# Moving the products of gates ("merges") of a gated linear attention from GpSimd to VectorE

## The reference

```python
# q, k, v, f_logit: (4 batches, 8 heads, 768 tokens, 48)
f = 1.0 / (1.0 + np.exp(-f_logit))
for t in range(S):
    state = f[:, :, t, :, None] * state + einsum('bhd,bhe->bhde', k[:, :, t], v[:, :, t])
    y[:, :, t] = einsum('bhd,bhde->bhe', q[:, :, t], state)
x = y as (3072 tokens, 384)
# first layer, w_in 384 x 2048, w_out 2048 x 384
h = x @ w_in
g = where(h >= 1, h, where(h <= -1, 0, (h + 1)**2 / 4))
x = g @ w_out
# second layer, w_gate and w_val 384 x 1536, w_out 1536 x 384
out = (silu(x @ w_gate) * (x @ w_val)) @ w_out
```

## Time and profile before

| | before |
|---|---|
| median of 3 runs | 1084.7 us (1084.14 to 1085.7) |
| profiled execution: its time | 1084.7 us |
| its span in the trace | 1082.9 us |
| PE busy | 1013.7 us, 94% |
| DVE busy | 539.7 us, 50% |
| ACT busy | 454.3 us, 42% |
| POOL busy | 449.7 us, 42% |
| POOL merges (L890) | 80 instructions, 44.1 us |

### The profile page before, as it was taken

How to read it: one execution, slowest core, us unless ns; L and a number is a source line. 1 busy time by engine, 2 the same in 40 slices (tenths; PEclk the granted TensorE clock), 3 DMA queues, 4 the chain that set the end, 5 groups by cost and what they waited for, 6 DMA issues and landing times.

```text
span 1082.9 us, 19234 instructions
## 1 busy us (share of the span) xinstructions
PE 1013.7 (94%) x7816; PEld 828.0 (76%) x7816; DVE 539.7 (50%) x743; ACT 454.3 (42%) x840; POOL 449.7 (42%) x368
## 2 busy tenths in 40 slices
PE   1484999999999999999999999999999999999997
PEld 1473778778777877877788888888888888888886
DVE  3965894885688388659736532222223222232221
ACT  6456647544753665375336532222122221222221
POOL 1856982764475366537526522212121221212121
PEclk9666999999999999999999999999999999999999
DMA  9323005202400600130043100010010010000000
GB/s 358 153 86 130 1 2 166 79 2 75 159 13 2 215 31 1 44 115 30 2 176 131 45 30 30 1 59 1 1 59 1 1 59 1 30 1 1 30 1 29
DMA packets 17367, 63.52 MB, mean 59 GB/s; under 512 B 1920, under 2 KB 2176, under 8 KB 16512
## 3 DMA queue, kind: packets, MB, share of 16 engines
q1 hardware_dynamic: 17280, 62.30, 15.9%
HBM read 52.85 MB, written 9.44 MB: 58 GB/s over the span
## 4 chain that ended last, share of the span: by engine, by line
PE 85%; issue 5%; ACT 4%; DVE 3%; POOL 2%; DMA 0%; POOLq 0%; ACTq 0%; SPq 0%; DVEq 0%
PE acc L447 11%; PE acc L448 10%; PE acc L449 10%; PE bank L474 7%; PE bank L473 7%; PE bank L475 7%; PE bank L346 6%; PE hid L433 6%; PE hid L434 5%; PE hid L435 5%; ACT scores L527 2%; PE hid L474 2%; PE hid L475 2%; PE hid L473 2%; PE bank L378 2%
## 5 line engine op out<-in xcount | busy, mean ns | idle before, releaser
L929 POOL TENSOR_TENSOR g_lo<-prod,g_hi 128x512 fp32r<-128x512 f32 x72 | 93.1, 1293 | 347.4 <-ACT g_hi L652 347.4
L922 POOL TENSOR_TENSOR g_lo<-act_tmp,g_hi 128x512 fp32r<-128x512 f32 x96 | 140.0, 1459 | 182.0 <-ACT g_hi L613 182.0
L827 DVE TENSOR_TENSOR sig<-sig,bank 128x512 f32<-128x512 f32 x72 | 49.5, 688 | 275.4 <-ACT sig L646 275.4
L740 DVE COPY_PREDICATED scores<-mask,bank 64x512 f32<-64x512 int32 x144 | 134.5, 934 | 32.7 <-PE bank L346 31.0
L652 ACT CAST g_hi<-prod 128x512 fp32r<-128x512 f32 x72 | 44.7, 621 | 247.8 <-PE acc L449 247.8
L433 PE MATMUL hid<-x_hi,win_hi 128*128 128x512 f32 x288 | 119.1, 414 | 16.1 <-DVE act_tmp L815 16.1
L882 POOL TENSOR_TENSOR keys<-keys,gates 128x512 f32<-128x512 f32 x82 | 108.0, 1317 | 57.5 <-PE bank L346 46.1
L613 ACT CAST g_hi<-act_tmp 128x512 fp32r<-128x512 f32 x96 | 59.5, 620 | 166.0 <-DVE act_tmp L815 166.0
L346 PEld LDWEIGHTS bank<-right_q,keys 128*64 128x64 f32 x2304 | 79.9, 148 | 62.4 <-issue 59.8
L346 PE MATMUL bank<-right_q,keys 128*64 128x64 f32 x2304 | 89.6, 236 | 39.6 <-ACT right_q L548 36.3
L447 PE MATMUL acc<-g_hi,wout_hi 128*128 128x512 f32 x288 | 116.9, 406 | 4.7 <-POOL g_lo L922 4.7
(11 more groups left out here) (79 smaller groups left out, 1858.7 us busy)
## 6 DMA issues: line engine op xcount, KB each, us to landing
gates<-in_f_dram SPq DMA_DIRECT2D x12, 512.0 KB, 5.4
queries<-in_q_dram SPq DMA_DIRECT2D x12, 512.0 KB, 4.9
keys<-in_k_dram SPq DMA_DIRECT2D x12, 512.0 KB, 4.8
values<-in_v_tok_dram SPq DMA_DIRECT2D x6, 1024.0 KB, 8.2
q_tok<-in_q_tok_dram SPq DMA_DIRECT2D x12, 384.0 KB, 8.1
k_tok<-in_k_tok_dram SPq DMA_DIRECT2D x12, 384.0 KB, 8.3
x_dram<-x_out SPq DMA_DIRECT2D x6, 768.0 KB, 3.2
x_raw<-x_dram SPq DMA_DIRECT2D x6, 768.0 KB, 5.5
```

The lines of the kernel that those rows point to most:

```text
L740: last = dve.copy_predicated(o, level_mask(li, half), t[rows(half), :].rearrange("p (x b r) -> p x b r", x=BP, r=m))
L922: pool.tensor_tensor(g_lo[:, c % RING, :], act_tmp[:, 2 + c % 2, :], g_hi[:, c % RING, :].bitcast(F32), ALU.subtract).then_inc(g_lo_done, 1)
```

## The change

`merge` moves from POOL to DVE. On DVE it stands directly ahead of `scale_q` of the step two later (`s >= 2`), the same group in the level above. The merges of the last level (only needed to decay the state, in units 1 to 4) stand ahead of `decay_state`. `scale_k` on POOL and `scale_q` on DVE wait for the same counter `g_merged` as before. `take_level` loses its wait for DVE's own take two steps earlier.

```diff
+        def merge(a, li, g):
+            s = 2 * li + g
+            dve.wait_ge(k_scaled, a * STEPS + s + 1)
+            dve.wait_ge(q_scaled, a * SCALED_A_UNIT + 2 + s + 1)
+            m = LEVELS[li]
+            left, right = (blocks(gates, li, g)[:, :, e, m - 1:m] for e in range(2))
+            dve.tensor_tensor(right, right, left, ALU.mult).then_inc(g_merged, 1)
...
             t = bank[fill(a, s) % 3]
-            if li:
-                dve.wait_ge(dve_took, a * DVE_A_UNIT + s - 1)
...
             for s in ladder(h):
+                if s >= 2:
+                    merge(a, s // 2 - 1, s % 2)
                 scale_q(a, s)
             if h == H_LAST_MERGE and 0 < a < UNITS - 1:
+                for g in range(2):
+                    merge(a, NL - 1, g)
                 decay_state(a)
...
-        def merge(a, s):
-            li, g = s // 2, s % 2
-            m = LEVELS[li]
-            pool.wait_ge(k_scaled, a * STEPS + s + 1)
-            pool.wait_ge(q_scaled, a * SCALED_A_UNIT + 2 + s + 1)
-            left, right = (blocks(gates, li, g)[:, :, e, m - 1:m] for e in range(2))
-            pool.tensor_tensor(right, right, left, ALU.mult).then_inc(g_merged, 1)
...
                 if s < STEPS - 2 or a < UNITS - 1:
                     scale_k(a, s)
-                if s < STEPS - 2 or 0 < a < UNITS - 1:
-                    merge(a, s)
```

## The result

The changed kernel takes **1100.3 us** (median of 4 runs, 1099.91 to 1100.85) where the kernel before took 1085.2 beside it (4 runs, 1084.14 to 1085.88): ratio 1.0141, 95% interval 1.0125 to 1.0156. It is slower, by 15.1 us where 7.6 were forecast. The profiled execution took 1098.95 us, its span is 1097.1, so 14.2 us more than before in both.

What follows compares the result with a forecast made beforehand. DVE was taken to bound unit 0, all three engines unit 1, TensorE units 2 to 5. Terms of 2.6, 1.0 and 4.0 us summed to +7.6 on 1084.7, so 1092.3 us, range 1085.5 to 1102.

Steps and rivals of the forecast that it cites:

- DVE sets ladder 0: Unit 0's 14 steps, run alone: DVE's program order sets their end, its time counts in full; DVE busy 41.3 of 44.0 us.
- The two exclude each other, and the splits then block the merges: Ladder 0: DVE and POOL products exclude each other; blocked time goes from 7.3 us to 4.9, mostly merges behind weight splits.
- DVE asks first: After each merge DVE asks in about 0.07 us, POOL in 0.14, so scale_q keeps its 0.69 us ahead of scale_k.
- The slip-in at steps 2 and 3: Units 2 to 5: POOL's L922 gets between merge and scale_q; activate comes late, TensorE stalls 1.0 us per unit.
- price of a merge on DVE: Twelve merges in each unit's ladder: 0.17 us fixed plus 1.02 ns per element, 4.06 us per unit, bounds 2 and 6.6.
- new wait: Each scale_q waits for the merge right ahead on DVE: 0.07 us per step, 0.9 us in ladder 0, bounds 0 and 0.15 per step.
- Ladder 0 by its own terms: Unit 0's sum: merges +4.06, hand-over +0.9, old blocked time −7.3, new blocked time +4.9, giving +2.6 us.
- Units 1 to 5: Ladders interleaved with the first feed-forward layer: +1.0 us for unit 1, +4.0 for units 2 to 5 together.
- The lead of TensorE: Units 2 to 5: activate was done 1.8 us before the hidden products needed it; a 2.8 us delay exceeds this by 1.0.
- Only ladder 0 and 1 pay: Rival, chance 0.21: in units 2 to 5 TensorE's lead of 1.8 us holds; 1088.3 us.
- POOL asks first: Rival, chance 0.09: scale_q of steps 2 to 13 stands behind scale_k; unit 0 loses 11.6 us, 1106 in all.
- Faster: Rival, chance 0.11: POOL's splits fall within the takes and miss the merges; ladder 0 gains 2.0 us, 1082 in all.

Runs made afterwards that it cites:

- e9: Changed kernel with seven of eight w_in weight splits moved on POOL out of ladder 0, behind unit 1's diagonal products: 1090.44 us, ratio 1.0054 to the kernel before.
- e1: Changed kernel with merges on DVE in unit 0 only, on POOL in the others, take_level's wait kept: 1088.87 us, ratio 1.0038 to the kernel before.
- e2: Changed kernel with merges on DVE in units 1 to 5 only, on POOL in unit 0, take_level's wait kept: 1093.18 us, ratio 1.0085 to the kernel before.
- e13: Kernel before with seven DVE products added at its very end, 256 or 64 elements at pitches 2 to 16; 256 elements at pitch 2 took 0.42 us.
- e15: Changed kernel with waits moved so that from step 2 on scale_q waits for the merge alone: 1094.12 us, ratio 1.0087 to the kernel before.
- e14: Changed kernel with merges of the same element counts but all at pitch 2, output not the reference's: 1093.89 us, ratio 1.0086 to the kernel before.
- e3: Changed kernel with take_level's dropped wait for DVE's own take two steps back restored: 1096.95 us, ratio 1.0117 to the kernel before.
- e10: Changed kernel with eight tiny memsets added at the start of DVE's list: 1096.6 us, ratio 1.0112 to the kernel before.
- e7: Changed kernel with scale_k on POOL waiting for scale_q of its own step in all units: 1099.69 us, ratio 1.014 to the kernel before.
- e12: Changed kernel with each merge one place earlier on DVE, ahead of the previous place's scale_q, take_level's wait kept: 1097.02 us, ratio 1.0113 to the kernel before.

## Why the prediction was right in sign and wrong in size

**Right.** *DVE sets ladder 0*: `scale_q` went down by 6.8 us and the ladder up by 3.9, as its list demands (its last `scale_q` starts at 70.16 us, before at 66.24), and TensorE's first outputs (L378) follow it, at 70.99 instead of 67.07. *The two exclude each other, and the splits then block the merges*: 4.5 us of blocked merges and 0.5 of blocked `scale_q` where 4.9 were laid out; in e9, with all but one split away, the merges are blocked for 0.3. *DVE asks first*, even at an equal recorded start. *The slip-in at steps 2 and 3 and one late `activate` near the seventh step* came in every unit from 2 on. e1 and e2 show that the two parts stand by themselves.

**The step that failed is "price of a merge on DVE", and with it the "new wait"**, both terms of the sum.

- Price: I took 0.17 us and 1.02 ns per element from products whose elements lie side by side. The bounds (2 to 6.6 us per unit) held the measured 4.8; the value taken, 4.06, was too low. From pitch 4 on an element costs about 1.8 ns (e13: 0.62 − 0.17 over 256), and every merge of a unit but its first two has such a pitch. The expression for `left` and `right`, one element out of every m, says so; I read only the count.
- Hand-over: 0.07 us forecast, 0.13 measured, within the bound of 0.15. It isn't the wait for the own result by itself, which is 0.03 to 0.04 in e13 and e15; with the other two waits taken from between the pair, it is gone.

Ladder 0 by its own terms: 4.8 + 12 × 0.13 − 7.3 + 5.0 = +4.1 us against 3.9 measured at the last `scale_q`; 2.6 was forecast. Of these 3.9 the hidden products see 3.1 to 3.8 in the two profiles.

*Units 1 to 5, the same two terms again.* Each unit has some 0.8 us of dearer merges and 0.7 of dearer hand-over. The lead of TensorE was used up in the forecast already, so that what is added shows in the stall: 1.6 us for 1.0 in units 2, 3 and 5, and 2.2 for 1.0 in unit 1. e14 brings units 2, 3 and 5 back to 1.0 or 1.1, e15 to 1.3 or 1.4.

*Unit 4, in nobody's list.* The halt, 0.35 us longer than the usual hand-over, POOL's instruction in it, and the loss of clock afterwards make 2.6 us of the miss of 7.5, more than half of it (1.6) the clock. e3 and e10, which lack it there, are 3.3 and 3.7 us faster than the changed kernel.

By the lag, the miss (14.3 against 7.6) is: ladder 0 0.5, unit 1 1.2, units 2, 3, 5 1.8, unit 4 3.2 (2.6 of it the halt and what follows), together 6.7. By the experiments it is about 2.7 for the price (e14), 1.4 for the hand-over (estimated from e15's 2.3: the forecast was 0.06 of its 0.10 us off) and 2.6 for the halt.

**The rivals.** *Only ladder 0 and 1 pay* fell: each unit pays. *POOL asks first* fell but for that one place; e7, without it, has unit 4 at 2.1 us instead of 4.2. *Faster* fell by its own condition, since the splits do meet the merges; e9 shows that even without them the change costs 13.7 us. The rule of the Trainium skill (GPSIMD Engine Reference, "Engine selection") that such work belongs on VectorE is no help where VectorE is the full engine: in ladder 0 DVE's time counts in full, and in units 2 to 5 POOL had more time free than DVE for the same merges. The Trainium skill's rule on shared ports (SBUF — State Buffer, "Who interferes with whom") agrees with the rows above, as where the merge at 47.09 has to wait for the split of 46.68.

**Open.** Why DVE halts just there: the halt moves with eight instructions put ahead (e10), goes with other waits (e3, e15), stays when POOL is held back (e7), and comes with a packet of instructions each time, but other such packets come without one. What made the clock fall isn't settled either. The wait of 2.2 us alone doesn't do it: e9 waits 2.24 us at the same place and keeps 1.00. Nothing else was tried on it.

## To carry to other kernels

Price a moved operation by its access pattern as well as its element count: a one-out-of-m slice is not a 512-element row. On the engine that sets the end, count each added pair of dependent instructions with its waits, and keep one wait, the one that ends last, directly ahead of the second. When a run comes out as forecast, look whether its parts do too: e9's 2 us were in another unit than expected. When two engines exclude each other, look first at which of the *other* engine's instructions could stand elsewhere: moving weight splits by a few lines gave 7.7 us and one wait over 2 us more, while moving the merges cost 15.

## What the runs showed of the hardware

- A product of DVE with two float32 inputs at pitch 2 takes 0.42 us for 256 elements, at pitch 4 0.62 and at pitch 8 0.67.
- Waiting for the engine's own last result: 0.03 to 0.04 us with one wait ahead of the instruction, 0.13 with three, though all three counters but one had long been reached.
- At equal recorded starts of a DVE and a POOL product DVE goes first (44.90 us above; the same at 41.92), and POOL's takes 1.82 us. A POOL product that was already waiting got in between two successive products of DVE (208.75, and 215.47 in e12).
- DVE halts for 0.48 us instead of 0.13 at one place of its list in the changed kernel, at another when eight instructions are added ahead. In all seven runs a packet of instructions of about 8 KB follows 0.6 to 0.7 us after the halt.
- TensorE's granted clock went from 1.00 (420 to 424 us) to 0.70 (424 to 428), a mean between its two levels, 1.2 and 2.4 GHz, after a wait of 2.2 us. After the same wait in e9 it stayed at 1.00, and the unit lost 1.6 us less.
